# A recurrence, a feed-forward block and top-2 experts on one core: the order of the seam, the place of the router steps, the size of a slot entry

## What is computed

```python
# 1. a linear recurrence, per batch and head
for t in range(S):
    cur = einsum('bhd,bhe->bhde', u * k[t], v[t])
    y[t] = einsum('bhd,bhde->bhe', r[t], state + cur)
    state = w[t][..., None] * state + einsum('bhd,bhe->bhde', k[t], v[t])
x = y as (3072, 384)
# 2. a gated feed-forward block
x = ((x @ w1) * (x @ w2) @ w3) @ w_out            # 384 -> 1024 -> 1024 -> 384
# 3. noisy top-2 routing to 8 experts
noisy = x @ w_gate + log1p(exp(x @ w_noise)) * noise
top2, weights = two largest of noisy, softmax over the two
out[token] = sum over its two experts e of weight * (relu(x @ ew1[e]) @ ew2[e])
```

## Time and profile before

| | |
|---|---|
| median of 3 executions | 1048.24 us (1047.87 to 1051.14) |
| the profiled execution | 1056.58 us, span of the trace 1054.9 us, clock 0.986 of full |
| TensorE busy | 998.7 us, 95% |
| VectorE, ScalarE, GpSimd busy | 687.9, 566.9, 218.4 us |
| recurrence and feed-forward | to about 540 us |
| expert visits | from about 539 us to the end |

### The profile page before, as it was taken

The page is one execution under the profiler, slowest core; times in us unless marked ns, Lnnn a source line. Parts: engine busy times, 40 slices in busy tenths (PEclk is TensorE's granted clock), DMA queues, the critical chain, the costliest instruction groups (busy, mean ns, idle before and its releaser), DMA issues.

```text
span 1054.9 us, 18983 instructions
## 1 busy us (share of the span) xinstructions
PE 998.7 (95%) x7177; PEld 942.0 (89%) x7177; DVE 687.9 (65%) x1151; ACT 566.9 (54%) x1034; POOL 218.4 (21%) x210
## 2 busy tenths in 40 slices
PE   6999999999999899999795999999999999999995
PEld 4766999888999898899695999999999999999995
DVE  5887776868685776443674657575775857476570
ACT  4666455445463555342452557575665756566471
POOL 0000000020202020112125232333234233323321
PEclk9999999999999999999898999999999999999998
DMA  9664433264445533110766779787888978778861
GB/s 252 157 180 105 98 72 95 60 81 104 65 92 75 116 80 40 45 51 1 262 130 132 212 198 299 213 251 227 241 258 218 296 210 253 244 225 269 225 158 16
DMA packets 189215, 166.32 MB, mean 158 GB/s; under 512 B 118130, under 2 KB 172788, under 8 KB 189124
## 3 DMA queue, kind: packets, MB, share of 16 engines
q1 hardware_dynamic: 175348, 144.76, 50.7%
q0 software_dynamic: 12976, 20.32, 9.5%
q10 hardware_dynamic: 800, 0.02, 0.0%
HBM read 141.21 MB, written 25.22 MB: 158 GB/s over the span
## 4 chain that ended last, share of the span: by engine, by line
PE 46%; DMA 3%; DVE 2%; POOL 1%; ACT 1%; issue 1%; SPq 0%; POOLq 0%; DVEq 0%; ACTq 0%
PE pp L1254 18%; PE bank L1238 18%; PE yu L1297 3%; PE tr L1219 2%; PE yu L1279 1%; PE fx L1279 1%; DMA tokens<-ffn_out,who 1%; DMA slot_entry<-entry,slot_i 1%; PE bank L829 1%; POOL slot_entry L999 1%; PE tr L1288 1%; PE fx L812 0%; PE fx L829 0%; DMA up_raw<-in_moe_w 0%; DVE set_up_l L1326 0%
## 5 line engine op out<-in xcount | busy, mean ns | idle before, releaser
L1147 POOL DMA_INDIRECT result<-x2s,who x55 | 92.7, 1686 | 300.1 <-ACT x2s L1371 281.1
L1358 DVE SCALAR_TENSOR_TENSOR abl<-bank,abh 128x512 fp32r<-128x512 f32 x96 | 66.2, 690 | 111.3 <-ACT abh L1353 111.3
L999 POOL DMA_INDIRECT slot_entry<-entry,slot_i x48 | 50.7, 1056 | 378.5 <-DVE token_f L988 366.3
L1238 PE MATMUL bank<-xh,set_up_h 128*128 128x256 f32 x384 | 109.2, 284 | 0.0
L1238 PE MATMUL bank<-xl,set_up_h 128*128 128x256 f32 x384 | 108.6, 283 | 0.0
L1238 PE MATMUL bank<-xh,set_up_l 128*128 128x256 f32 x384 | 108.6, 283 | 0.0
L1353 ACT ACTIVATE abh<-bank 128x512 fp32r<-128x512 f32 x96 | 57.4, 598 | 81.7 <-PE bank L1238 81.5
L812 PE MATMUL bank<-xh,w12h 128*128 128x384 f32 x264 | 93.3, 354 | 6.8 <-DVE work L897 5.4
L812 PE MATMUL bank<-xl,w12h 128*128 128x384 f32 x264 | 89.5, 339 | 1.6 <-issue 1.6
L812 PE MATMUL bank<-xh,w12l 128*128 128x384 f32 x264 | 89.6, 339 | 0.0
L1254 PE MATMUL pp<-set_down_h,abh 128*128 128x384 f32 x256 | 87.7, 343 | 0.0
(11 more groups left out here) (263 smaller groups left out, 2815.0 us busy)
## 6 DMA issues: line engine op xcount, KB each, us to landing
up_raw<-in_moe_w SPq DMA_DIRECT2D x93, 512.0 KB, 4.5
down_raw<-in_moe_w SPq DMA_DIRECT2D x124, 384.0 KB, 5.0
padded<-in_w SPq DMA_DIRECT2D x32, 144.0 KB, 2.7
padded<-in_k SPq DMA_DIRECT2D x32, 144.0 KB, 2.8
padded<-in_r SPq DMA_DIRECT2D x32, 144.0 KB, 2.8
vs<-in_v SPq DMA_DIRECT2D x32, 144.0 KB, 2.8
attention_out<-yt SPq DMA_DIRECT2D x64, 72.0 KB, 1.9
tokens<-attention_out SPq DMA_DIRECT2D x8, 576.0 KB, 4.2
```

Source lines behind the costliest of these rows:

```text
L999: nc.gpsimd.indirect_dma_start(slot_entry, bass.IndirectOffsetOnAxis(slot_i[:, s, n:n + 1], 0), entry[:, s, n, :], None).then_inc(scattere ...
L1147: nc.gpsimd.indirect_dma_start(out, bass.IndirectOffsetOnAxis(who[v % 4][:, s, 0:1], 0), yo[v % 2][:, s, 0:DM], None, bounds_check=N - 1, ...
L1238: last = nc.tensor.matmul(bank[m % 2][:, f * T2:(f + 1) * T2], wp[:, kk, c:c + P], xp[:, kk, :], start=(n == 0), stop=(n == 3 * KD - 1))
L1358: nc.vector.scalar_tensor_tensor(hl[:, 2 * m:2 * m + 2, :].rearrange("p a t -> p (a t)"), bank[m % 2][:, :], 0.0, hh[:, 2 * m:2 * m + 2, : ...
```

## The change

Four things are changed. (1) SyncE's order in the seam: the three up pieces of the first visit's weights come ahead of the rows of visits 0 and 1, the four down pieces behind them; the wait for the table moves along. (2) GpSimd's order: the gather of visit 2 comes ahead of the scatters of the last group. (3) `ROUTE_AT` goes from (4, 8, 10, 12) to (5, 9, 11, 13), and in `pair_slots` the queries step gets a slot of its own, one later than the keys. (4) An entry of `slot_entry` has 16 words (64 bytes) instead of 2; the words behind the second are zero. The table is filled at the start with 25088 such entries instead of 24832 of 8 bytes, `entry` is cleared once, and the read of `who` takes the first two words of each. Three small buffers share memory to make room.

```diff
+WORDS = 16
+PADS = 14
+SLOTS = P * PADS * PADS
-    slot_entry = nc.dram_tensor("slot_entry", [E * N + T2, 2], i32, kind="Internal").ap()
+    slot_entry = nc.dram_tensor("slot_entry", [SLOTS, WORDS], i32, kind="Internal").ap()
...
-                     [("derive", q + 1, 3)], [("derive", q + 1, 4), ("derive", q + 1, 5)], [], []]
+                     [("derive", q + 1, 3)], [("derive", q + 1, 4)], [("derive", q + 1, 5)], []]
...
-            pads = psb("pads", [P, (E * N + T2) // P // 2, 2], i32)
+            pads = psb("pads", [P, PADS, WORDS], i32)
...
-                            sp.dma_start(slot_entry.rearrange("(h p n) o -> p h (n o)", h=2, p=P),
-                                         pads[:, :, :].rearrange("p n o -> p (n o)").rearrange("p (h x) -> p h x", h=1)
-                                         .broadcast_to([P, 2, (E * N + T2) // P])).then_inc(pads_stored, 16)
+                            sp.dma_start(slot_entry.rearrange("(p a n) o -> p a (n o)", p=P, a=PADS),
+                                         pads[:, :, :].rearrange("p n o -> p (n o)").rearrange("p (a x) -> p a x", a=1)
+                                         .broadcast_to([P, PADS, PADS * WORDS])).then_inc(pads_stored, 16)
...
-            entry = psb("entry", [P, ST, 2, 2], i32)
+            entry = psb("entry", [P, ST, 2, WORDS], i32)
...
+                if i == 0:
+                    dve.wait_ge(entry_clear, 1)
...
-            ROUTE_AT = (4, 8, 10, 12)
+            ROUTE_AT = (5, 9, 11, 13)
...
                 if v == 0:
-                    sp.wait_ge(tables_ready, 1)
                     sp.wait_ge(scattered, 32 * ST * (GROUPS - NG))
...
-                sp.dma_start(who[v % 4][:, 0:n, :], slot_entry[bass.ds(t * P, n * P), :].rearrange("(p s) o -> p s o", s=n)
+                sp.dma_start(who[v % 4][:, 0:n, :], slot_entry[bass.ds(t * P, n * P), 0:2].rearrange("(p s) o -> p s o", s=n)
...
-            def sp_weights(sp, v):
-
+            def sp_weights(sp, v, lo=0, hi=7):
+
+                if v == 0 and lo == 0:
+                    sp.wait_ge(tables_ready, 1)
...
-                for n in range(7):
+                for n in range(lo, hi):
...
+                sp_weights(sp, 0, 0, KD)
                 sp_rows(sp, 0)
-                sp_weights(sp, 0)
-                for v in range(1, EARLY):
+                sp_rows(sp, 1)
+                sp_weights(sp, 0, KD, 7)
+                for v in range(2, EARLY):
                     sp_rows(sp, v)
...
+                nc.gpsimd.memset(entry[:, :, :, :], 0).then_inc(entry_clear, 1)
...
                 for q in range(NG):
+                    if q == NG - 1:
+                        pool_gather(pool, 2)
                     pool_scatter(pool, B - 1, q)
                 for v in range(NV):
-                    if v + 2 < NV:
+                    if 0 < v < NV - 2:
                         pool_gather(pool, v + 2)
                     pool_add(pool, v)
```

More of the change, by code:

```diff
@@ L35 @@
 TAIL = 3
+WORDS = 16
+PADS = 14
+SLOTS = P * PADS * PADS
+assert SLOTS >= E * N + T2
 LENGTH = {"up": 6, "down": 6, "turn": 0, "route": 0, "place": 0,
@@ L618, in first_pool @@
                 nc.gpsimd.memset(zeros[:, :], 0.0).then_inc(zeros_ready, 1)
-                nc.gpsimd.memset(pads[:, :, 1:2], 0)
+                nc.gpsimd.memset(pads[:, :, 1:WORDS], 0)
                 nc.gpsimd.memset(pads[:, :, 0:1], N).then_inc(pads_ready, 1)
@@ L747, in program @@
             over = flat_work[:, F2 + NL * 2 * E:F2 + NL * 2 * E + E * BPE].rearrange("p (e c) -> p e c", e=E)
-            place_j, moved_j, exp_j, block_j = psb("place_j", [P, NL]), psb("moved_j", [P, NL]), psb("exp_j", [P, NL]), psb("block_j", [P, NL])
+            place_j, moved_j = psb("place_j", [P, NL]), psb("moved_j", [P, NL])
+            exp_j = moved_j
+            block_j = flat_work[:, 5 * TG - NL:5 * TG]
             xr_loaded += [psem(f"xr_loaded{i}") for i in range(1, NG)]
@@ L1000, in pool_scatter @@
                                                      entry[:, s, n, :], None).then_inc(scattered, 16)
-            chosen_step, place_step = psem("chosen_step"), psem("place_step")
-            ROUTE_AT = (4, 8, 10, 12)
+            chosen_step, place_step, entry_clear = psem("chosen_step"), psem("place_step"), psem("entry_clear")
+            ROUTE_AT = (5, 9, 11, 13)
             TURN_AT = 4
```

## The result

The changed kernel takes 1019.5 us (1019.05 to 1019.79), the kernel before 1048.05 beside it: 28.5 us less by the medians. The ratio is 0.9723, interval 0.9702 to 0.9744. Its profiled execution took 1019.79 us with a span of 1018.1; against the profiled one of before that is 36.8 us less.

A forecast was written before the change was run, and what follows sets the result against it. TensorE, busy 95% of the span, bounds the kernel, so only its stalls can go: 8.9+12.9+5.4+6.6 = 33.8 us off the profiled 1056.58 gives 1022.8; allowing for the lower median (1014.4 to near 1020), 1016, range 1008 to 1028.

The forecast's parts named there:

- Route, 5.4 us: Route behind the product and queries one slot later end five TensorE waits of 1.08 us on VectorE's product: 5.4 us.
- the five waits: TensorE's waits of 1.08 us for a feed-forward product, once per group with route threaded in; all taken as gone.
- First seam stall, 8.9 us: At the seam to the experts, earlier first weights remove a 6.44 us wait and 2.5 us of slow clock.
- Second, 12.9: Gathering visit 2's tokens ahead of the last scatters removes 11.3 us of TensorE waiting and 1.6 of slow clock.
- Entries, 6.6 us: 64-byte entries end the scatter backlog, removing TensorE's waits at 227.0, 345.5 and 405.7: 6.6 us.
- the three waits: TensorE's waits of 1.62, 2.99 and 1.97 us at 227.0, 345.5 and 405.7, after scatter bursts.
- code that arrives late: Reading of ScalarE's 6.7 us wait for something "remote" in the backlog: instructions delivered late.
- the second of the two cases I named: If profiling makes code arrive late, the 6.6 us are partly not there to win: near 1020.
- (a): Rival: entries drain no faster, 6.6 us less gain and +1 for the down weights: 1024; chance 0.22.
- (b): Rival: the seam stalls again, for visit 3's tokens or weights: 8 us, 1024, or 1030 with (a); chance 0.17.
- (c): Rival: slower than before, as a 64-byte row costs more than 8 bytes and the drain grows; chance 0.03.
- (d): Rival: the waits named aren't the real ones, time within 0.3% of before; chance 0.02.

The follow-up runs named there:

- the third group: Runs on another chip: changed kernel again 1023.5 us, with 32-byte entries 1025.2, with 16-byte entries 1024.4; kernel before with the route change alone 1035.7.

## Why the prediction was right, and where not

Forecast 1016, range 1008 to 1028, measured 1019.5.

*Route, 5.4 us:* the five waits are gone, as said. The term was a little small: undoing it costs 5.9 us of span, 4.6 of them ahead of the sixth burst and 1.5 in the seam, and 6 to 8 in time. What I missed is the sixth place, in the seam, where I had kept only 0.4 for waits behind splits; the stall ahead of it had covered it.

*First seam stall, 8.9 us:* 8.4 by the traces, of which 1.5 come only with the new route places. *Second, 12.9:* 13.0. The mechanisms were right, and so was the slow clock as a part of each: the clock is 1.00 where it was 0.67 and 0.65. *What moves where:* the first weights leave at 469.73 and visit 3's second gather at 545.54; with the 15.4 us gained ahead of the seam added that is 485.1 and 560.9, where I had 485.2 and "near 560".

*Entries, 6.6 us:* the waits of the earlier trace rows are gone from the trace, and the drain fell from 10 to about 3.5 us (the 4.7 to the read of `who`, less 1.1). The term that a kernel shows which undoes this part alone is 3.9 us and not 6.6, with one of the three waits back. Of the premise, "a write of part of a unit" that "eight neighbours share", the first half by itself does nothing: 8 bytes in a row of 64 drain like 64. The row I took as the nearest, pieces of 768 bytes, could not tell. I also gave the three waits an end 9 to 12 us behind the last scatter; the one at 345.5 ends 13.2 behind it. And the step "code that arrives late" in such a backlog was too simple. Waits of the same kind, 3 us long, came in kernels without a backlog, the changed one among them. With the backlog they are longer (up to 7.7 us of ScalarE's time, against 3.2 at most), but it isn't their only cause. That it is code stays an inference: no run names the releaser.

*The sum:* 33.8 predicted, 36.8 in the profiled executions. The missing 3 us are ahead of the sixth burst (15.4 against 12.0). There TensorE is idle 11.5 us less and busy 3.9 us less. Of the latter 1.3 is its slow clock behind the wait at 345.5, which I had not added; the rest isn't traced to a cause. The windows view of before and after (the same instants, not the same work):

```profile
340.00:350.00 10.00, 7.01 (x44) 6.25 (x44) 7.36 (x16) 4.24 (x11) 0.00 (x0) 0.83 0.56 61
```
```profile
340.00:350.00 10.00, 10.00 (x78) 9.76 (x76) 8.28 (x12) 7.20 (x18) 0.00 (x0) 1.00 0.39 100
```

*From the profiled execution to the median:* 28.5 of 36.8 remain. The profiled execution before was 8.3 us above its median, after it is level. By its number that is the second of the two cases I named (near 1020), but not by its reason: the kernel with 8-byte entries and both new orders has its profiled execution (1023.6) within its others, so profiling by itself isn't what makes the waits. None of the 8.3 us had to be taken off: 1056.58 less 36.8 is 1019.8. I took 6.8 off (1022.8 to 1016). The step that failed is that choice; the sum that was 3 us too small hid nearly half of it, so that the forecast came to within 3.5 us partly by luck. The kernel before spreads over 1042.8 to 1060.1 in all its runs here, within one group over 4 to 10 us, and the changed kernel over 0.7 and 1.8 within its groups. My guess is that a slow execution of before is one in which the backlog fell badly, so that its stalls can't all be taken off the median; with one trace of that kernel it isn't shown.

*The rivals:* (a), a drain no faster, is refuted; the rule of the Trainium skill that spoke for it ("DMA: Bandwidth & Descriptors", Specifications: below 512 bytes the engine does a read-modify-write) may hold, but it doesn't set the drain here, as 8 bytes in rows of 64 drain like 64. (b) did not come: neither trace of the changed kernel has a stall for visit 3's tokens or for weights. What cost 4 us near 540 in the third group is the wait for something remote, which no rival named. (c) is refuted: a row costs less. The filling of the table (1568 KB, landed 7.7 us after its issue) lengthened no wait of TensorE between 55 and 85 us (one of 1.04 us there, 1.03 before). (d) is refuted by the waits that went.

*What the prediction did not say* is that its terms overlap. It priced each part at what it removes from the kernel before, and for this pair of kernels the sum is right. But the parts are two covers for one thing: with large entries the first weights are in time even behind them (order worth 0.7 us), and the gather is late by 4 us rather than 11 (worth 5.7). With 8-byte entries the orders are worth 4 to 7 and 10 to 13. A reader who took the list of terms as the worth of each edit would keep SyncE's reordering, which with large entries buys next to nothing.

## What to carry to other kernels

A list that a scatter writes in small entries side by side was slow to drain here, and the transfers behind it paid; give each entry a row of its own (here the drain behind rows of 32 bytes was as short as behind 64) before reordering queues around the delay. When two edits aim at the same stall, price each with the other in place as well: the sum can be right while the terms are not. And where the profiled execution lies well above its median, ask which of its stalls the other executions have too before taking them off the median.

## What I had not expected of the hardware

A burst of six scatters of 128 eight-byte entries side by side holds back the transfers behind it: 20 to 43 GB/s in the 10 us that begin 1 us after its last issue, against 168 and 176 with the same eight bytes spread to rows of 64. Of the first weights issued into that drain the three pieces took 9.0 us to land (the median), with large entries 4.3. They seem to lengthen the drain in turn: with 8-byte entries 12.4 and 13.7 us from the last scatter's issue to the read of `who` with them ahead, 9.0, 9.1 and 11.3 without; with rows of 64, 4.6 and 4.7 against 3.2. And an unchanged kernel can differ by 4 us from one group of runs to the next, with a wait for something that no engine of the core releases and a slow clock behind it.
